# Low-weight half products of neighbouring first-layer blocks on the array's two row halves, with reordered opening transfers and other banks for the last sums

## What is computed

```
for t in range(768):                       # 2 batches, 8 heads, head size 40
    C = f_stab * C + i_stab * outer(v_t, k_t)
    n = f_stab * n + i_stab * k_t
    y_t = sigmoid(o_t) * (C @ q_t) / max(|n . q_t|, 1)
x = y as 1536 tokens of 320 values
p = domain_probs / sum(domain_probs)
for e in range(4):                         # w1[e] is 320 x 1024, w2[e] is 1024 x 320
    h = max(x @ w1[e], 0)
    out += p[:, e] * (h @ w2[e])
```

## Time and profile before

| | |
|---|---|
| runs | 3 |
| median | 407.63 us |
| lowest and highest | 406.55, 408.7 us |
| the profiled execution, its own time | 409.92 us |
| span of its instructions | 408.0 us |
| granted clock, mean | 0.995 |
| PE busy | 402.0 us, 99% |
| DVE, ACT, POOL busy | 263.5, 192.4, 193.7 us |

### The profile page before, as it was taken

How to read it: one execution, slowest core, us unless ns; L and a number is a source line. 1 busy time by engine, 2 the same in 40 slices (tenths; PEclk the granted TensorE clock), 3 DMA queues, 4 the chain that set the end, 5 groups by cost and what they waited for, 6 DMA issues and landing times.

```text
span 408.0 us, 7284 instructions
## 1 busy us (share of the span) xinstructions
PE 402.0 (99%) x2650; PEld 388.7 (95%) x2650; DVE 263.5 (65%) x490; ACT 192.4 (47%) x378; POOL 193.7 (47%) x227
## 2 busy tenths in 40 slices
PE   8999999999999999999999999999999999999997
PEld 8898999999999999999999999889899989999996
DVE  6873966786465555475259893677666666667653
ACT  5583647845264478444116433353454345434420
POOL 5854843476053889832502001568435553556300
PEclk9998999999999999999999999999999999999999
DMA  7889909878263585261025002222112211230002
GB/s 275 278 280 382 372 35 292 328 260 277 96 227 104 181 258 199 82 212 48 2 49 123 0 2 84 86 72 98 31 54 84 85 42 43 84 102 17 0 2 96
DMA packets 18052, 54.48 MB, mean 134 GB/s; under 512 B 2177, under 2 KB 8850, under 8 KB 16866
## 3 DMA queue, kind: packets, MB, share of 16 engines
q1 hardware_dynamic: 17442, 52.63, 38.0%
q10 hardware_dynamic: 576, 1.40, 1.0%
HBM read 50.40 MB, written 2.05 MB: 129 GB/s over the span
## 4 chain that ended last, share of the span: by engine, by line
PE 92%; DMA 3%; DVE 1%; SPq 1%; POOL 1%; issue 0%; ACT 0%; DVEq 0%
PE acc_ps L1641 21%; PE hid_ps L1622 21%; PE acc_ps L1707 15%; PE out_ps L1578 4%; PE hid_ps L1707 3%; DMA w_raw<-in_w_b 3%; PE out_ps L1683 2%; PE out_ps L1684 2%; PE out_ps L1686 2%; PE out_ps L1685 2%; PE acc_ps L1622 2%; PE score_ps L1522 2%; PE out_ps L1585 2%; PE add_ps L1683 1%; PE add_ps L1684 1%; PE score_ps L1684 1%
## 5 line engine op out<-in xcount | busy, mean ns | idle before, releaser
L1165 DVE SCALAR_TENSOR_TENSOR h_lo<-hid_ps,h_hi 128x384 fp32r<-128x384 f32 (+1 forms) x72 | 36.8, 512 | 79.5 <-ACT h_hi L821 79.2
L821 ACT ACTIVATE h_hi<-hid_ps 128x384 fp32r<-128x384 f32 (+1 forms) x72 | 32.8, 455 | 106.2 <-PE hid_ps L1622 106.0
L1641 PE MATMUL acc_ps<-w_hi,h_hi 128*128 128x320 f32 x208 | 66.3, 319 | 0.0
L1641 PE MATMUL acc_ps<-w_hi,h_lo 128*128 128x320 f32 x208 | 64.2, 309 | 0.0
L1641 PE MATMUL acc_ps<-w_lo,h_hi 128*128 128x320 f32 x208 | 64.0, 308 | 0.0
L1622 PE MATMUL hid_ps<-xt_hi,w_hi 128*128 128x384 f32 (+1 forms) x216 | 58.0, 323 | 0.1
L1622 PE MATMUL hid_ps<-xt_hi,w_lo 128*128 128x384 f32 (+1 forms) x216 | 57.6, 320 | 0.4 <-POOL w_lo L624 0.4
L624 POOL TENSOR_TENSOR w_lo<-w_raw,w_hi 128x384 fp32r<-128x384 f32 x40 | 43.4, 1088 | 19.1 <-ACT w_hi L807 19.1
L694 POOL TENSOR_TENSOR w_hi<-w_raw,w_hi 128x640 fp32r<-128x640 f32 x12 | 19.5, 1623 | 51.7 <-ACT w_hi L864 51.7
L1641 PEld LDWEIGHTS acc_ps<-w_hi,h_hi 128*128 128x128 f32 x208 | 39.4, 189 | 0.2
L598 POOL TENSOR_SCALAR_AFFINE_SELECT dec_w<-dec_w 128x512 f32<-128x512 f32 x22 | 14.9, 678 | 51.8 <-ACT dec_w L786 51.8
(11 more groups left out here) (251 smaller groups left out, 994.0 us busy)
## 6 DMA issues: line engine op xcount, KB each, us to landing
w_raw<-in_w_b SPq DMA_DIRECT2D x19, 704.0 KB, 7.3
w_raw<-in_w_s SPq DMA_DIRECT2D x12, 832.0 KB, 4.6
raw<-in_qk_s SPq DMA_DIRECT2D x8, 1024.0 KB
g_all<-g_dram SPq DMA_DIRECT2D x10, 512.0 KB, 6.2
kv<-in_kv_n SPq DMA_DIRECT2D x12, 352.0 KB, 6.0
q_pack<-in_q_p SPq DMA_DIRECT2D x10, 192.0 KB, 6.4
out_y<-y_acc SPq DMA_DIRECT2D x12, 160.0 KB, 1.8
carry<-g_dram SPq DMA_DIRECT2D x30, 60.0 KB
```

The costliest lines, as they stand in the source:

```text
L821: nc.scalar.activation(h_hi[:, M % RING, 0:cols], hid_bank(M)[:, 0:cols], ACT.Relu).then_inc(hid_hi, 1)
L1165: nc.vector.scalar_tensor_tensor(h_lo[:, M % RING, 0:cols], hid_bank(M)[:, 0:cols], 0.0, h_hi[:, M % RING, 0:cols].bitcast(fp32), ALU.max, ...
L1641: last = nc.tensor.matmul(acc_ps[t][:, 0:DM], x, w, start=(f == 0 and i == 0), stop=(f == NF - 1 and i == 2))
```

## The change

There are four edits.

1. **Pairs.** From slot 16 on, `up(M)` of an even M makes only seven matmuls by itself. As its eighth it takes the low weights by the high inputs alone (partitions 64 to 127), and right behind it puts the same product of block M + 1 (partitions 0 to 63, in the other block's bank, which this begins). `up(M + 1)` then has seven matmuls. For this the high inputs are needed on partitions 0 to 63 as well: `xt_again(k)` on ACT copies them to `xt_top`, once for each unit. The pair waits for the next block's bank and low weights. The size of a buffer for descriptors is set, which leaves room for `xt_top`.
2. **Opening transfers.** On SP the loads of the weight pairs 3, 4 and 5 stand earlier.
3. **Banks of the last sums.** The second half's sums of steps 10 and 11 go to `late_acc`.
4. **Order of the last turns.** In the loop's step 12 the second half's turns of step 10 come before the first half's of step 11.

```diff
+AGAIN_TOP, TWO_FROM = 6, 16
+def two_at_once(M):
+    return M >= TWO_FROM and M % 2 == 0
+def begins_bank(M):
+    return M < TWO_FROM or M % 2 == 0
+LATE_FREED = max(wide_evictions(p, 1, PAIRS - 1) for p in range(1, STEPS, 2) if pairs(p) == PAIRS)
...
+        late_acc = [hid_ps[0], score_ps, out_ps]
+        def sum_bank(half, p, i):
+            return late_acc[i] if half == 1 and p >= STEPS - 2 else wide_acc[i]
...
             load_g(2)
+            load_pair(sp, 3)
             sp.wait_ge(out_done, 1)
             sp.wait_ge(add_done, 1)
             load_kv(sp, 2)
             load_carry(2)
-            load_pair(sp, 3)
+            load_pair(sp, 4)
             load_g(3)
             reload_scores(3)
+            load_pair(sp, 5)
             sp.wait_ge(out_done, 2)
             sp.wait_ge(add_done, 2)
             load_kv(sp, 3)
             load_carry(3)
-            load_pair(sp, 4)
-            load_pair(sp, 5)
             load_pair(sp, 6)
...
+            def xt_again(k):
+                act.wait_ge(xt_hi_done, k + 1)
+                tok = slice(k * L, (k + 1) * L)
+                nc.scalar.activation(xt_top[:, tok], xt_hi[64:128, 2, tok], ACT.Copy).then_inc(xt_top_done, 1)
...
             split_high(2, None)
+            xt_again(0)
+            xt_again(1)
             split_high(3, None)
...
+                if (k := unit_at(M, AGAIN_TOP)) is not None:
+                    xt_again(k)
...
-                terms += [(hi[:, 2, :], xt_hi[:, 2, tok]), (lo[:, 2, :], xt_hi[:, 2, tok])]
+                terms += [(hi[:, 2, :], xt_hi[:, 2, tok])]
+                if M < TWO_FROM:
+                    terms += [(lo[:, 2, :], xt_hi[:, 2, tok])]
...
+                if two_at_once(M):
+                    wait_if(pe, hid_lo, hid_free(M + 1))
+                    if first_of_load(M):
+                        pe.wait_ge(w_lo_done, NF * load + f + 2)
+                    if f == 0 or M == TWO_FROM:
+                        pe.wait_ge(xt_top_done, first + tiles)
+                    last = nc.tensor.matmul(hid_bank(M)[:, 0:tiles * L], lo[64:128, 2, :], xt_hi[64:128, 2, tok], start=False, stop=True)
+                    nc.tensor.matmul(hid_bank(M + 1)[:, 0:tiles * L], w_lo[0:64, f + 1, 256:384], xt_top[:, tok], start=True, stop=False)
                 last.then_inc(hid_ready, 1)
...
+                    elif half == 1 and p == STEPS - 2:
+                        if i == 0:
+                            pe.wait_ge(acc_free, LATE_FREED)
+                        else:
+                            pe.wait_ge(low_of[(0, 11, 21)[i]], STEPS)
...
-                ahead, behind = halves_of(t)
+                ahead, behind = halves_of(t) if t != STEPS else halves_of(t)[::-1]
...
+    nc = _bacc.Bacc("TRN2", target_bir_lowering=False, num_devices=1, dynamic_dma_scratch_size=8192)
```

More of the change, by code:

```diff
@@ L266, in build @@
         xt_hi, xt_lo = sb("xt_hi", [128, 3, NT * L], f32r), sb("xt_lo", [128, 2, NT * L], f32r)
+        xt_top = sb("xt_top", [DM - 256, NT * L], f32r)
         w_hi, w_lo = sb("w_hi", [128, NF, WB], f32r), sb("w_lo", [128, NF, WB], f32r)
@@ L340, in build @@
         gated = sem("gated")
-        x_ready, xt_ps, xt_hi_done, xt_done = sem("x_ready"), sem("xt_ps"), sem("xt_hi_done"), sem("xt_done")
+        x_ready, xt_ps, xt_hi_done, xt_done, xt_top_done = (
+            sem("x_ready"), sem("xt_ps"), sem("xt_hi_done"), sem("xt_done"), sem("xt_top_done"))
         w_hi_done, w_lo_done, w_dn_done = sem("w_hi_done"), sem("w_lo_done"), sem("w_dn_done")
@@ L1344, in add_wide @@
                 share = pn[:, n, EXPERTS[2 * p // NF]:EXPERTS[2 * p // NF] + 1]
-                nc.vector.scalar_tensor_tensor(y_acc[:, n, :], wide_acc[i][:, 0:DM], share, y_acc[:, n, :],
+                nc.vector.scalar_tensor_tensor(y_acc[:, n, :], sum_bank(half, p, i)[:, 0:DM], share, y_acc[:, n, :],
                                                ALU.mult, ALU.add).then_inc(acc_free, 1)
@@ L1621, in up @@
                         pe.wait_ge(xt_done, first + tiles)
-                    last = nc.tensor.matmul(hid_bank(M)[:, 0:tiles * L], w, x, start=(i == 0),
-                                            stop=(i == len(terms) - 1))
+                    last = nc.tensor.matmul(hid_bank(M)[:, 0:tiles * L], w, x, start=(i == 0 and begins_bank(M)),
+                                            stop=(i == len(terms) - 1 and not two_at_once(M)))
+                if two_at_once(M):
[6 more added lines that the diff above has]
+                    nc.tensor.matmul(hid_bank(M + 1)[:, 0:tiles * L], w_lo[0:64, f + 1, 256:384], xt_top[:, tok], start=True, stop=False)
                 last.then_inc(hid_ready, 1)
@@ L1706, in wide_down @@
                     for j, (x, w) in enumerate(((hi, w_1), (hi, w_2), (lo, w_1))):
-                        last = nc.tensor.matmul(wide_acc[i][:, 0:DM], x, w, start=(p % 2 == 0 and f == 0 and j == 0),
+                        last = nc.tensor.matmul(sum_bank(half, p, i)[:, 0:DM], x, w, start=(p % 2 == 0 and f == 0 and j == 0),
                                                 stop=(p % 2 == 1 and f == 1 and j == 2))
@@ L1829 @@
     }
-    nc = _bacc.Bacc("TRN2", target_bir_lowering=False, num_devices=1)
+    nc = _bacc.Bacc("TRN2", target_bir_lowering=False, num_devices=1, dynamic_dma_scratch_size=8192)
     maps, args = {}, []
```

## The result

| | forecast | measured |
|---|---|---|
| time, median | 410.9 us (404.5 to 414.0) | **414.48 us** (414.15 to 415.12, 4 runs) |
| before, in the same comparison | | 407.59 us (406.55 to 408.7, 4 runs) |
| ratio | 1.008 | **1.0163**, 95% interval 1.0144 to 1.0183 |
| pairs in place of full matmuls | +6.4 us | +7.4 us, from the rows below |
| end | -0.4 us | the step is gone; -0.5 us by two medians (e6, e7) |

A forecast was written before the change was run, and what follows sets the result against it. The PE's matmuls were taken as the bound; pairs +6.4, copies +0.1, opening -3.4, end -0.4 made +2.7 us, 412.6 profiled. With the median 2.3 lower, cases of 410.3 and 412.0 led to 410.9 us, range 404.5 to 414.0.

The forecast's parts named there:

- What bounds the kernel: The PE, busy 402.0 of 408.0 us: matmul time added or removed goes into the span, except in a few holes.
- The pairs: Slots 16 to 79, 32 pairs: two tile-size changes each, 0.19 us per change; +6.4 us in all, bounds +5.1 to +7.7.
- The saving: In the pairs, two half products streaming together in place of two full matmuls: 5.2 us at most.
- New waits and copies: Pairs' waits for the next block's bank and low weights cost nothing; ACT's 12 short copies cost +0.1 us.
- The end: Second half's last sums, whose first matmul starts 0.47 us behind its neighbour, find their banks ready: -0.4 us.
- The opening: Earlier weight pairs 3 and 4 remove PE stalls and the fallen clock: -3.4 us profiled, -2.8 us at the median.
- Same gain: Case for the median: the opening regains as much as in the profiled execution, giving 410.3 us.
- gain of 1.7 only: Case for the median: an unprofiled opening stalls less, so less is regained, giving 412.0 us.
- the clock's 1.7 us: Opening: 3.5 us at half clock, from 38.6 to 42.1 us, counted as 1.7 us of the loss to regain.
- pair 4's two stalls: Opening: PE waits for pair 4's high weights (0.22 idle) and low weights (0.58), with 0.2 us more counted for each.
- pair 3's 0.64 us: Opening: the PE's stall for weight pair 3 at 29.87 us, 0.44 us, with 0.2 more counted.
- the opening isn't regained: Rival: the moved transfers and unit 3's data stall attention or drop the clock again; 413.8 us, chance 0.12.

The follow-up runs named there:

- e6: The kernel before with only the new order of SP's opening weight transfers; 407.69 us, ratio 0.9991.
- e7: The kernel before with the new opening order, new banks and new order of last turns, without pairs or copies; 407.22 us, ratio 0.998.
- e1: The changed kernel without any pairs; copies, new transfer order and end stay; 407.25 us, ratio 0.9983.
- e3: The changed kernel with both half products over all 128 rows, in the same places and behind the same waits; 407.24 us, ratio 0.9986.
- e2: The changed kernel with the old transfer order, banks and last turns, so pairs and copies alone; 415.36 us, ratio 1.018.
- e4: The changed kernel with the second half product also on rows 64 to 127, so the two can't run together; 419.96 us, ratio 1.0294.
- e5: The kernel before, unchanged, run and profiled again as a kernel of its own; 408.09 us, ratio 1.0002.
- e9: e7 with the load of weight pair 3 moved further ahead on SP, right behind q of unit 2; 408.47 us, ratio 1.0002.
- e10: e7 with the load of weight pair 3 issued from ACT's queue, right behind pair 2; 408.40 us, ratio 1.0003.

## Why the prediction was half right

**What bounds the kernel: right.** The PE's row of matmuls is the bound in the middle, and what is put into it is in the span: with no idle time in either, 7.4 us in the rows of the pairs and 7.2 us between the medians of the changed kernel and e1.

**The pairs: mechanism right, size off by 1.0 us.** "A change thus costs 0.09 + 0.10 = 0.19 us", both parts at each of the 64 changes, is nearly what the rows show, and e3 takes all of it away by the tile's height alone. The saving was right too (e4: 5.5 us against 5.2 at most). The term that was mis-sized is the working of one pair, "0.16 streaming, 0.19 change, 0.17 for both half products, 0.19 change = 0.71". In the three pieces that the timeline shows, that was 0.25 to the first load, 0.36 from there to the load of `down`, and its bare 0.10; measured are 0.27, 0.37 and 0.10 (0.25 less 0.147). Both bare loads were right, and the drain with what streams ahead of it is 0.01 to 0.02 longer at each change. 0.03 is little beside one pair and 1.0 us over 32; 0.219 and 0.265 instead of 0.185 and 0.24 make 7.4 us, within the bounds of 5.1 to 7.7; by medians it is 7.2 (against e1) and 7.5 (e2 against before).

The Trainium skill, "TensorEngine Tiling (Array Packing)", Key Properties, with its drain at a mode switch, is what the traces bear out. The Trainium skill, "TensorE: Matmul & The Clock Gate", Part 3, is right within the pack, since the two start within 0.01 us and end as one. By itself it would have given -5 us where +7.4 was measured.

**New waits and copies: right.** None of the PE's waits in the profile after is new, and e3, which keeps them all, costs nothing.

**The end: right.** The step of 0.47 us is 0.18 now; -0.4 was forecast, and -0.5 lies between the medians of e6 and e7, which alone would not be clear of noise.

**The opening: this is the step that failed**, in "I take -3.4 for the profiled execution" and, above all, in the way from there to the median, "Same gain: 410.3; gain of 1.7 only: 412.0. I say 410.9". The reading of the profiled execution was sound: the changed kernel's profile has none of those stalls. By the start of slot 12 it is 2.15 us ahead of the first profile (50.45 against 52.60 us), though it began its real work later: the 24 matmuls with which the PE starts took longer. The first pieces of the two chains show it, the changed kernel's here, before's 4.54 us for the same 24:

```profile
1.15 5.49 PE hid_ps L1502 x24
```

Without those 0.95 us the opening would have gained 3.1. (+7.4 - 3.1 + 0.95 - 0.4 = 4.85 us, where the spans differ by 4.5.) But a PE that stands at pair 4 and a clock of 0.51 aren't the kernel's habit. Of 84 further executions of before whose clock is listed (74 beside the other runs and e5's 10), three had a mean granted clock below 0.998 (0.996; 408.48, 408.64 and 410.03 us), and the one profile of an ordinary execution (e5) has neither. e6, with the new order alone, gains 0.4 us at the median and at most 0.9 by its interval. The median never lost those 3.4 us, so nothing could give them back. An ordinary execution does lose something: 1.5 us at 27 to 31 us in e5's profile, 1.3 of it behind pair 3. With the new order no profile has a wait for pair 3's transfer, yet the median gains 0.4 only. In e7's and e3's profiles weights are late all the same, behind ACT's wait for `g_all`; how much of the 1.3 us that takes back at the median isn't shown.

The prediction did see that "the median of the runs shown is 2.3 lower" and that "then there is less to regain". It took only the clock's 1.7 us out for that case, kept the stalls, and gave that case the smaller part of the weight. What was measured for this term is 0.4 us in place of 2.8. Without the clock and without pair 4's two stalls (0.42 and 0.78) its own sum leaves pair 3's 0.64 us, and the median shows 0.4. The rival "the opening isn't regained", 413.8 us, was the nearest to what came, for another reason than it gave: no transfers collide in the profile after; there is little to regain. Either miss alone would have left the time within the range: 411.9 us with the pairs' 1.0 more, 413.3 with the opening's 2.4. So from the median of 407.6: +7.4 for the pairs, -0.4 for the opening, -0.5 for the end make 414.1, and 414.5 was measured. The other 0.4 lies within what medians of four runs tell.

**Open.** What starts the bad opening in some executions (the same program, the same order) wasn't settled. One rival stands untested, that the profiler itself, or being the first execution, favours it. With the old order of transfers two of the three profiled executions have the fallen clock (before and e2, not e5), and of the 88 others whose clock is listed only three have a mean below 0.998. If so, a profile shows stalls that other executions don't have. Neither was it settled what e9 and e10 lose.

## What to carry to other kernels

Two half-height matmuls side by side save one matmul, but in a dense stream a trip into another tile size and back costs 0.219 + 0.175 = 0.39 us, more than two matmuls of 384 columns: count the trips, and pack only where more than that is saved on each.

If the profiled execution lies above the median, don't promise its stalls to the median: a second profile of the unchanged kernel (e5) and one run of the single edit (e6) showed that most of the 3.4 us to be regained are usually not lost. The same holds for a profile taken to explain a loss, as e9's.

Asking for a transfer earlier need not help: e9 and e10 asked for pair 3 much earlier and lost e7's gain. Where an engine works in order, look first at what it waits for ahead of the late work, here `g_all`, 1.35 us in e7's profile.

## What the runs showed of the hardware

- The cost of a change of tile size is paid twice each time, and the second part stands one matmul later than one looks for it: after the way in, the load comes 0.27 us behind the start of a matmul of 384 columns (0.175 is the rule); after the way out, `down`'s second matmul comes 0.25 behind its first (0.15 is the rule).
- The array's two row halves do run at once with fp32r operands, 384 columns each from two different sources into two different banks: starts within 0.01 us, 0.44 and 0.43 long. On one half, one behind the other, the same products make the kernel 5.5 us longer (e4).
- The start of a kernel varies by up to 1 us from one execution to the next. The same 24 opening matmuls took 4.54 and 5.49 us: their pace rises from 6 or 7 in a microsecond to 9, in the first profile of before at 4 to 5 us, in the changed kernel's not before 7 us, while the clock column shows 1.00 throughout.
- In e9 holes of 0.9 and 0.6 us in the PE's stream near 30 us stood ahead of a granted clock of 0.75 and 0.88 in the two windows there, that is, 1.2 GHz from 31 to 34 us and 2.4 GHz behind it; in e5 holes of 0.3 and 0.6 us at the same place stood ahead of no fall.
